# An attention, MoE and Mish kernel: the second head's key hash placed ahead of the third tile, rounding and scaling moved to GpSimd, the first queries loaded over two queues

## The reference

```
q_bits = (q @ proj > 0);  k_bits = (k @ proj > 0)          # 6 bits, 8 heads, 768 tokens, 64 columns
mask   = bucket(q_bits)[:, None] == bucket(k_bits)[None, :]
scores = where(mask, q @ k.T / 8, -1e9)
attn   = exp(scores - max);  attn /= sum(attn) + 1e-9;  x = attn @ v
x      = top-1 mixture of 8 experts with capacity 192 (512 -> 1024, relu, -> 512), scaled by the gate
h      = x @ w_in;  g = h * tanh(softplus(h));  out = g @ w_out         # 512 -> 2048 -> 512
```

## Time and profile before

| | us |
|---|---|
| median of 3 runs | 410.65 (410.51 to 410.78) |
| the profiled execution | 414.38 |
| its span on the core | 412.6 |
| TensorE busy | 399.7 |
| VectorE busy | 250.4 |
| ScalarE busy | 202.1 |
| GpSimd busy | 80.7 |

### The profile page before, as it was taken

One profiled execution on the slowest core, in us unless ns is written; L12 is line 12 of the kernel. 1 busy time (PEld: TensorE's weight loads), 2 busy tenths in 40 slices (PEclk: granted clock), 3 DMA queues, 4 the chain that ended last, 5 costly groups with the idle time before them and its releaser, 6 DMA issues.

```text
span 412.6 us, 7248 instructions
## 1 busy us (share of the span) xinstructions
PE 399.7 (97%) x2667; PEld 366.6 (89%) x2668; DVE 250.4 (61%) x441; ACT 202.1 (49%) x389; POOL 80.7 (20%) x81
## 2 busy tenths in 40 slices
PE   7999999999999999999999999999999999999995
PEld 3578998998999879899999999999988999899984
DVE  3698889899899561311011111118899998877761
ACT  5778977977788520301101111117667555553541
POOL 0640320330510032274742700000000000000005
PEclk9799999999999999999999999999999999999999
DMA  8492941891700044999899999800000000000003
GB/s 297 169 217 72 264 100 40 268 228 44 252 3 0 2 155 143 414 400 367 309 390 373 346 375 390 313 2 0 2 0 2 1 1 2 0 2 0 0 2 153
DMA packets 15595, 62.85 MB, mean 152 GB/s; under 512 B 2896, under 2 KB 3536, under 8 KB 11344
## 3 DMA queue, kind: packets, MB, share of 16 engines
q1 hardware_dynamic: 14176, 58.51, 41.6%
q0 software_dynamic: 960, 3.15, 2.0%
q10 hardware_dynamic: 432, 0.83, 0.6%
HBM read 49.89 MB, written 3.15 MB: 129 GB/s over the span
## 4 chain that ended last, share of the span: by engine, by line
PE 69%; DVE 13%; ACT 7%; DMA 5%; issue 2%; POOL 2%; POOLq 0%; ACTq 0%; SPq 0%; DVEq 0%
PE ps L727 13%; PE ps L830 12%; PE ps L745 12%; PE ps L805 12%; PE ps L659 5%; PE ps L632 5%; PE ps L545 4%; DVE ptl L1192 3%; DVE nmax L1135 3%; PE ps L615 2%; DMA xg<-rows 2%; ACT prob L915 2%; PE ps L508 2%; ACT pth L953 1%; DMA qq<-in_first 1%
## 5 line engine op out<-in xcount | busy, mean ns | idle before, releaser
L727 PE MATMUL ps<-xs,ring 128*128 x512 | 60.0, 277 | 0.1
L727 PEld LDWEIGHTS ps<-xs,ring 128*128 128x128 f32 x512 | 58.7, 192 | 0.8 <-issue 0.5
L745 PE MATMUL ps<-hs,ring 128*128 128x128 f32 (+1 forms) x512 | 59.2, 276 | 0.0
L745 PEld LDWEIGHTS ps<-hs,ring 128*128 128x128 f32 x512 | 58.5, 192 | 0.0
L1192 DVE TENSOR_TENSOR ptl<-ps,pth 128x384 fp32r<-128x384 f32 x96 | 48.8, 550 | 4.5 <-ACT pth L953 4.4
L953 ACT ACTIVATE pth<-ps 128x384 fp32r<-128x384 f32 x96 | 42.2, 495 | 18.3 <-PE ps L659 17.6
L1135 DVE TENSOR_REDUCE nmax<-ps 128x1 f32<-128x768 f32 x48 | 45.8, 955 | 6.6 <-PE ps L545 5.6
L545 PE MATMUL ps<-ops 128*128 128x384 f32 x192 | 45.8, 361 | 0.8 <-ACT prob L915 0.8
L915 ACT ACTIVATE prob<-ps,nmax 128x768 f32<-128x768 f32 x48 | 43.5, 907 | 3.9 <-DVE nmax L1135 3.9
L805 PE MATMUL ps<-yh,wih 128*128 128x384 f32 x128 | 43.0, 336 | 0.3 <-ACT hc L1036 0.3
L659 PE MATMUL ps<-cfs,prob 128*128 128x128 f32 x288 | 41.5, 277 | 1.9 <-DVE ptl L1192 1.6
(11 more groups left out here) (161 smaller groups left out, 655.7 us busy)
## 6 DMA issues: line engine op xcount, KB each, us to landing
ring<-in_w SPq DMA_DIRECT2D x32, 1024.0 KB, 6.9
winraw<-in_w_in SPq DMA_DIRECT2D x8, 512.0 KB, 6.3
woutraw<-in_w_out SPq DMA_DIRECT2D x8, 512.0 KB
ops<-kh SPq DMA_DIRECT2D x12, 192.0 KB, 3.8
ops<-qh SPq DMA_DIRECT2D x6, 384.0 KB, 6.4
xg<-rows SPq DMA_DIRECT2D x1, 1539.0 KB, 6.9
raw<-in_vt SPq DMA_DIRECT2D x4, 384.0 KB, 5.6
raw<-in_qt SPq DMA_DIRECT2D x3, 384.0 KB, 6.8
```

Of the source, the lines that this page charges most:

```text
L727: last = mm(ps[:, fc // 2, (fc % 2) * WIDE:(fc % 2) * WIDE + W], wa[:, 2 * fc // KF, kd, P * (fc % (KF // 2)):P * (fc % (KF // 2)) + P], x ...
L745: last = mm(ps[:, 4 + half * KD // 2 + k, 0:W], wb[:, half, fc, P * k:P * k + P], hs[:, fc, 0:W], start=(fc == 0), stop=(fc == KF - 1))
```

## The change

What it does, part by part:

- The second head's hash is cut in two functions. `hash_keys(1)` stands behind the scores of tile 1, `hash_queries(1)` where the whole hash stood. Two filler matmuls stand between the first head's two halves.
- GpSimd takes over the unsplit query copies of both heads, the second head's query scaling and query remainder (ScalarE only casts that head's queries), and for the later pairs the two casts and the scaling.
- The tasks of pair 1 stand one step later.
- Partitions 96 to 127 of the first head's queries are loaded by SP behind the first keys, the other 96 by ScalarE.

The diff, cut to its core:

```diff
+        EDGE = 96
-        TASKS = {("B", 3): (1, 0), ("A", 4): (1, 1), ("B", 4): (1, 2), ("B", 5): (1, 3),
-                 ("A", 6): (1, 4), ("B", 6): (1, 5)}
+        TASKS = {("B", 4): (1, 0), ("A", 5): (1, 1), ("B", 5): (1, 2), ("B", 6): (1, 3),
+                 ("A", 7): (1, 4), ("B", 7): (1, 5)}
...
             load_head(0)
+            sp.dma_start(early["qq"][EDGE:P, 0, :], first[0, 1, EDGE:P, :]).then_inc(s["q0"], 16)
             sp.dma_start(cbs[:, 0:heads_to], cb[:, 0:heads_to]).then_inc(s["c"], 16)
...
             def split_kq(g):
-                hold(gp, s["passed_gp"], s["ka"], 2 * g - 1)
+                hold(gp, s["passed_gp"], s[f"rk{g % 2}"], 32 * ((g + 1) // 2))
+                hold(gp, s["passed_gp"], s["opsA"], DMASA * (g - 1))
+                hold(gp, s["passed_gp"], s["pd"], PD * (g - 1))
+                nc.gpsimd.tensor_copy(kh, rk[0]).then_inc(s["ka"], 1)
+                nc.gpsimd.tensor_scalar(rk[1], rk[1], SCALE, None, ALU.mult).then_inc(s["ks"], 1)
+                hold(gp, s["passed_gp"], s["ks"], g)
+                nc.gpsimd.tensor_copy(qh, rk[1]).then_inc(s["ka"], 1)
+                hold(gp, s["passed_gp"], s["ka"], 2 * g)
                 nc.gpsimd.tensor_tensor(kl, rk[0], kh, sub).then_inc(s["kl"], 1)
-                hold(gp, s["passed_gp"], s["ka"], 2 * g)
                 nc.gpsimd.tensor_tensor(ql, rk[1], qh, sub).then_inc(s["kl"], 1)
+            def q_copy(p, cs):
+                nc.gpsimd.tensor_scalar(ops[0:D, p, QA, cs], early["qq"][0:D, p, cs], SCALE, None,
+                                        ALU.mult).then_inc(s["ch"], 1)
+            hold(gp, s["passed_gp"], s["q0"], 32)
+            for c in range(2):
+                q_copy(0, slice(c * HALF, c * HALF + HALF))
+            hold(gp, s["passed_gp"], s["q1"], 16)
+            nc.gpsimd.tensor_scalar(early["qq"][:, 1, :], early["qq"][:, 1, :], SCALE, None, ALU.mult).then_inc(s["qs"], 1)
+            hold(gp, s["passed_gp"], s["qs"], 1)
+            nc.gpsimd.tensor_copy(ops[0:D, 1, QA, :], early["qq"][0:D, 1, :]).then_inc(s["ch"], 1)
             hold(gp, s["passed_gp"], s["ca"], 5)
             nc.gpsimd.tensor_tensor(ops[0:D, 1, KB, :], early["kk"][0:D, 1, :], ops[0:D, 1, KA, :],
                                     sub).then_inc(s["cp"], 1)
+            hold(gp, s["passed_gp"], s["ca"], 6)
+            nc.gpsimd.tensor_tensor(ops[D:P, 1, QA, :], early["qq"][D:P, 1, :], ops[D:P, 1, QB, :],
+                                    sub).then_inc(s["cl"], 1)
+            hold(gp, s["passed_gp"], s["cl"], 1)
...
-            def head_hash(p, banks):
+            def hash_keys(p, banks):
...
+            def hash_queries(p, banks):
...
                 for c in range(2):
-                    pe.wait_ge(s["cq"], (c + 3, 5)[p])
+                    pe.wait_ge(s["cl" if p else "cq"], (c + 3, 1)[p])
...
-            head_hash(0, (4, 5))
+            hash_keys(0, (4, 5))
+            keep_clock(2, 0)
+            hash_queries(0, (4, 5))
...
             scores(1)
+            hash_keys(1, (XB, OB))
...
-                        head_hash(1, (XB, OB))
+                        hash_queries(1, (XB, OB))
...
-            for p in range(2):
-                act.dma_start(early["qq"][:, p, :], first[p, 1, :, :]).then_inc(s[f"q{p}"], 16)
+            act.dma_start(early["qq"][0:EDGE, 0, :], first[0, 1, 0:EDGE, :]).then_inc(s["q0"], 16)
+            act.dma_start(early["qq"][:, 1, :], first[1, 1, :, :]).then_inc(s["q1"], 16)
...
-                av(ops[0:D, p, QA, cs], early["qq"][0:D, p, cs], ACT.Copy, scale=SCALE).then_inc(s["ch"], 1)
...
-            act.wait_ge(s["q1"], 16)
-            q_high(1, slice(0, T))
-
-            def pair_high(g, part):
...
+            act.wait_ge(s["qs"], 1)
+            av(ops[:, 1, QB, :], early["qq"][:, 1, :], ACT.Copy).then_inc(s["ca"], 1)
...
-            dve.wait_ge(s["ca"], 6)
-            q_low(1, slice(0, T))
```

29 lines of the change are left out of this document (5 added, 24 removed).

## The result

The changed kernel takes **411.77 us** (median of 16 runs, 411.43 to 412.76). The kernel before, run beside it, takes 410.74 us (16 runs, 410.26 to 413.42). The ratio is 1.0024, with a 95% interval of 1.0015 to 1.0034: the change makes the kernel slower, by 0.15 to 0.34%. The prediction was 406.9 with a range to 410.2.

What follows compares the result with a forecast made beforehand. The prediction took TensorE, busy 97% of the span, to bound the kernel. Gains of 3.08 (opening), 0.45 (key hash) and 0.2 us (pairs' rounding) sum to 3.73, taking 410.65 to 406.9, range 405.9 to 410.2.

Steps and rivals of the forecast that it cites:

- The clock: Opening: a denser TensorE keeps the granted clock full from 9.2 to 16 us, gaining 2.72 us.
- plain runs never have the fall: Rival: only the profiled execution has the half clock in the opening, so the time is 409.6; chance 0.14.
- the two signs named for the opening: First row maximum near 11.7 us with full clock from 9.2 to 16; ScalarE's first query operation before 6.5.
- Queries over two queues: First loads: splitting the first head's queries over two queues lands them 0.17 us earlier, bounds nothing to 0.52.
- Unsplit copies to GpSimd: Opening: GpSimd's two 64x384 copies take 0.45 us each, so ScalarE's second high part directly follows the first.
- Two fillers ahead of the queries: Opening: two filler matmuls at full clock end at 7.26 us, before the first remainder's 7.5, costing nothing.
- Second head's key hash: Moved ahead of the third tile's scores into TensorE's wait: gains 0.45 us, bounds 0 and 0.84.
- The gap itself: TensorE's wait ahead of tile 2's scores, 1.5 us, holds the 0.85 us key hash with a wait left behind.
- Pairs' rounding on GpSimd: Later pairs: relieving ScalarE gains 0.2 us, bounds 0 and 0.35; five tiles of pair 3 in 13.5 us.
- GpSimd is late: Rival: second head's queries or pair 1's parts come 1 to 1.5 us beyond the cover, giving 408.2; chance 0.08.
- the third term: Rounding of the later pairs moved off ScalarE: 0.16 us on the path for pair 3, 0.2 in all.
- The slower rival: Tiles 1 to 4: a thinner TensorE loses the clock later, costing 3.1 us, giving 412.9; chance 0.08.

Runs made afterwards that it cites:

- b_again: The kernel before, unchanged, run and profiled again; 411.08 us, ratio 1.0006.
- e_hash_only: The kernel before with only the second head's key hash moved ahead of the third tile; 410.63 us, ratio 1.0001.
- e_pe_only: The kernel before with only the split query load, the two fillers and the moved key hash, nothing moved to GpSimd; 410.62 us, ratio 0.9993.
- e_move_noadd: The kernel before with the moved key hash and without VectorE's addition of 1e-9, nothing new on GpSimd; 407.65 us, ratio 0.9933.
- e_cast: The changed kernel with GpSimd's scalings written as plain casts, so scores are not scaled by 1/8; 409.98 us, ratio 0.9978.
- e_open_back: The changed kernel with the first two heads' query work back on ScalarE and VectorE, tasks still one step later; 411.37 us, ratio 1.0002.
- e_best_add: The kernel before with the moved key hash and the later pairs' two roundings on GpSimd, addition of 1e-9 kept; 409.92 us, ratio 0.9981.
- e_best: The kernel before with the moved key hash, the later pairs' two roundings on GpSimd, and no addition of 1e-9; 409.40 us, ratio 0.9959.
- e_noadd: The changed kernel without VectorE's addition of 1e-9 to the row sums; 409.45 us, ratio 0.9971.
- e_b_noadd: The kernel before without VectorE's addition of 1e-9 to the row sums; 408.53 us, ratio 0.9949.
- e_copies_only: The kernel before with only the first head's two scaled query copies moved to GpSimd; 411.62 us, ratio 1.0029.

## Why the prediction was wrong, point by point

**The clock: the step that failed first.** 2.72 of the 3.73 us rested on one execution whose granted clock had fallen at 9.2 us. The prediction named the rival (plain runs never have the fall) and the evidence for it: the profiled execution was 3.7 us above the median. It set the rival at a chance of 0.14 with "nothing but the profile shows the clock". That evidence should have decided, since the three plain runs lay within 0.27 us of each other and 3.6 us below the profiled one. Had they had the fall too, nothing would have been left to explain those 3.6 us; the other kernels' profiled executions lie within 1.1 us of their plain runs' median. All 19 traces taken since have the clock at its full level there. The same execution had its queries late as well, at 6.54 us where b_again has 5.23. So the two signs named for the opening proved little: the first row maximum came at 12.17 us, ahead of 14.73 but behind b_again's 11.33 (11.65 was forecast), and the first query operation came "before 6.5" in every other trace, with the split or without.

**Queries over two queues: wrong sign.** Forecast 0.17 us earlier; measured about 0.5 later at the landing, and in the plain runs nothing that can be told (e_hash_only with one transfer and e_pe_only with two: 410.63 and 410.62). The bound "nothing" was one-sided without a reason. The rule of the Trainium skill's page "DMA: Bandwidth & Descriptors", section "Rules for kernel authors", that the prediction quotes, by which such a split gains nothing, was nearer; that it loses is what these traces add.

**Unsplit copies to GpSimd: the price of the term.** Forecast 0.45 us each, upper bound the two-input price (0.92 for 384 elements); measured 1.21 to 1.24, above the bound. In the changed kernel TensorE waits 0.56 us for the second copy, and tile 0 starts 0.96 us later than in e_pe_only, which differs only in work given to GpSimd. I had two prices of GpSimd and took it that a multiplication with one input must lie between them. The Trainium skill's page "GPSIMD Engine Reference", section "Engine selection", puts one-input work at roughly line rate. The cast of 128x768 in 0.82 us may be that; the scaling of the same elements takes 2.13 us, more than two inputs do (1.83), and there the measurement decides.

**Two fillers ahead of the queries: free, but pointless.** They were meant to keep a clock that the median never loses. e_hash_only, without them and without the split, takes as long as e_pe_only with them.

**Second head's key hash: the size right, the place not.** 0.45 forecast; 0.35 measured from tile 2 to tile 5 in e_pe_only and in e_hash_only (and 0.36 in e_move_noadd, from -0.23 to -0.59), after 1.0 at tile 3. The reason was half right. The rest was to be lost in VectorE's queue, at pair 1's bits and matches by tile 10; it is gone by tile 5. In e_hash_only TensorE waits 0.51 us ahead of the transposes at 19.27 for VectorE's remainder, which itself has waited 0.43 us for ScalarE, busy with pair 1's scaling and rounding from 16.51 to 18.26. That the number fits is partly luck. The gap itself was there: in the changed kernel 0.24 us of wait is left behind the moved matmuls, at 14.21.

**Pairs' rounding on GpSimd: three errors.** (a) GpSimd's lateness. Ready at 24.0 or 25.5 was forecast for pair 1; it was 27.38, behind 2.42 + 2.12 us of scaling in the opening and 2.13 more for the pair. From tile 5 to 12 the changed kernel loses 1.31 us; e_cast, with all else the same, 0.15. This is the rival "GpSimd is late", with the size that it was given (1 to 1.5). (b) The addition, which the prediction did not have. Where `ql` is early enough (e_open_back), VectorE's addition meets GpSimd's subtraction for 1.47 us, and the loss is the same, 1.46 us from tile 5 to 12; that the addition makes it is shown by e_best_add against e_best, where one meeting costs 1.35. Where `ql` is late, taking the addition away gains little (1.09 us lost in e_noadd), and only with neither in the way does the loss shrink (0.15 in e_cast; e_best gains 0.19). (c) The gain itself. Five tiles of pair 3 were to take 13.5 us; they take 13.72 (71.24 to 84.96), against 13.65 in b_again (70.33 to 83.98). The relief is there: the step to tile 28 is 3.25 us instead of 3.79. But it comes from an addition that is no longer stretched at 79.0, because GpSimd's subtractions now lie earlier; and the steps to tiles 25 and 26 grow by 0.46 and 0.32, because the addition at 72.20 takes 1.81 us instead of 0.16. The wait moved, it did not go. Without any addition the same five tiles take 12.84 in e_noadd (70.41 to 83.25) and 12.98 in e_b_noadd (68.95 to 81.93): there the rounding and scaling on GpSimd are worth 0.14, as the third term had it (0.16). In e_best, where the 128x48 addition is met, they take 13.42.

**The sum.** By the changed kernel's line of the table: +0.85 in the opening (the copies' price, less an e_pe_only that lies at -0.11), -1.00 at tile 3 (the key hash), +0.11 to tile 5 (the queues' taking back, less ScalarE's relief), +1.31 to tile 12 (`ql` late), -0.37 at pair 2, +0.08 at pair 3, -0.08 up to tile 47: +0.90 against b_again. Behind tile 47, where nothing differs, the changed kernel's execution is 0.44 us longer than b_again's; over all traces that part varies from 278.31 to 279.29 us. The medians, run side by side, have +1.03. The prediction's rivals were taken one at a time; what came was two of them together ("plain runs never have the fall" and "GpSimd is late") plus a price beyond its bound. The slower rival that was named, a clock lost later, did not happen. (The lower end of the range is a slip: 406.9 less 0.35, 0.39 and 0.15 is 406.0, not 405.9.)

## What to carry to other kernels

Before a term is built on a profile, set the profiled execution beside the plain runs: if it is longer by as much as the term is worth, the term is probably a property of that one execution. Price an operation by a row of that same operation on that same engine; two other prices are no bounds. And before moving work to GpSimd, look in VectorE's rows for small instructions whose duration varies (0.16 here and 0.68 there, in the kernel before already), and for small ones that are about to meet GpSimd's new work: they mark the places where the two engines shut each other out, and taking such an instruction away was worth more than all parts of this change.

## What the runs showed of the hardware

- **GpSimd's multiplication by a constant is the dearest of its operations here for its size**: 2.13 us for 128x768 in fp32, 1.21 to 1.24 for 64x384; a copy or a cast 0.83, a subtraction of two tensors 1.83.
- **VectorE's addition of a constant within SBUF waits for the GpSimd instruction under way**: 128x3 elements take 0.16 us alone and up to 1.83 us beside a subtraction (1.84), a cast (0.48) or a memset (0.82, in b_again, ending at 111.19 where the memset ends at 111.17). A reduce of the same elements takes 0.15 beside the same subtraction. The addition of two tensors of 128x48 takes 0.20 us alone and 0.96 to 1.04 beside a subtraction (e_best, e_best_add). It goes the other way too: GpSimd's cast of 128x768 takes 1.56 us in b_again, where VectorE's remainder with two SBUF inputs is under way, instead of 0.82.
- **Not everything shuts out**: beside GpSimd's slow scaling (6.04 to 8.46 in the changed kernel) VectorE's two remainders took 0.60 and 0.55 us, hardly more than the 0.55 they take alone; in e_cast, beside a cast and a copy, the second took 1.63. Why the scaling lets them pass wasn't tried.
- **A reciprocal is not stretched, but what waits for it can start late**: in e_b_noadd it takes 0.17 us at 108.13, and the next instruction starts 0.44 us behind its end, while a memset runs on GpSimd until 108.93. What lies behind it is open.
- **The granted clock fell to its half level in one execution of the kernel before and in no other profiled one**, for the same instructions: its mean is 0.991 over that execution and 0.997 to 1.000 over the 19 others. Among the plain runs only e_copies_only (three of ten, 0.991 to 0.996) and e_hash_only (one of twelve, 0.994) have lower means, and these are their slowest. What set it off is open.
